# First batch reordered: queries load first, attention runs in a row, products of theta with the token weights' transposes between them

## The reference, cut to what matters

```
# attention without softmax: 8 batches, 8 heads, 576 tokens, head size 64
kv  = k^T v                                   # per head, 64 x 64
x   = rmsnorm(q @ kv) * g_norm                # -> [8, 576, 512], token-major
# first block
theta = x @ w_theta                           # 512 x 512
y   = w_tok_r @ (x*cos(theta)) + w_tok_i @ (x*sin(theta))    # 576 x 576 weights
u   = x + y
x2  = u + relu(u @ w_ch)
# second block
u2  = x2 + (relu(x2^T @ w_tok1) @ w_tok2)^T
out = u2 + relu(u2 @ w_ch1) @ w_ch2
```

## Time and profile before

| | us |
|---|---|
| median of 3 runs | 1176.14 (1175.67 to 1176.28) |
| profiled execution, device time | 1176.91 |
| its span in the profile | 1175.1 |
| PE busy | 1154.3 (98%) |
| DVE busy | 834.9 (71%) |
| ACT busy | 481.0 (41%) |
| POOL busy | 327.9 (28%) |

### The profile page before, as it was taken

One profiled execution on the slowest core, in us unless ns is written; L12 is line 12 of the kernel. 1 busy time (PEld: TensorE's weight loads), 2 busy tenths in 40 slices (PEclk: granted clock), 3 DMA queues, 4 the chain that ended last, 5 costly groups with the idle time before them and its releaser, 6 DMA issues.

```text
span 1175.1 us, 20563 instructions
## 1 busy us (share of the span) xinstructions
PE 1154.3 (98%) x7790; PEld 1116.7 (95%) x7790; DVE 834.9 (71%) x1243; ACT 481.0 (41%) x758; POOL 327.9 (28%) x210
## 2 busy tenths in 40 slices
PE   5999999999999999999999999999999999999998
PEld 5799999999999999999988999999999999999998
DVE  3968878686969687777557667667666786666664
ACT  3623425141424233334343555555556543333331
POOL 4462434444353534331552313214200000000000
PEclk9999999999999999999999999999999999999999
DMA  9714526160625330319997888666768999999983
GB/s 278 197 28 107 122 69 133 44 144 13 164 38 149 52 80 0 83 42 303 332 310 279 280 310 272 266 238 242 286 229 312 397 300 293 262 252 307 296 207 54
DMA packets 327383, 228.25 MB, mean 194 GB/s; under 512 B 231440, under 2 KB 295312, under 8 KB 326288
## 3 DMA queue, kind: packets, MB, share of 16 engines
q1 hardware_dynamic: 324912, 227.03, 63.3%
q10 hardware_dynamic: 2400, 0.30, 0.2%
HBM read 136.84 MB, written 92.80 MB: 195 GB/s over the span
## 4 chain that ended last, share of the span: by engine, by line
PE 86%; DMA 5%; DVE 3%; SPq 2%; issue 1%; POOL 1%; ACT 1%; DVEq 0%; ACTq 0%; POOLq 0%
PE bank L43 10%; PE bank L45 10%; PE bank L44 10%; PE bank L1377 10%; PE bank L1379 10%; PE bank L1378 10%; PE bank L367 6%; PE bank L373 6%; PE bank L368 6%; DMA u_scratch<-attention_u 3%; PE bank L312 3%; PE bank L326 1%; PE bank L282 1%; DMA attention_g<-g_scratch 1%; DVE attention_u L1268 1%
## 5 line engine op out<-in xcount | busy, mean ns | idle before, releaser
L367 PE MATMUL bank<-weights_tok,z_z 128*128 128x288 f32 x576 | 164.3, 300 | 0.3
L368 PE MATMUL bank<-weights_tok,z_z 128*128 128x288 f32 x576 | 161.2, 294 | 0.0
L373 PE MATMUL bank<-weights_tok,z_z 128*128 128x288 f32 x576 | 125.0, 295 | 0.8 <-POOL z_z L965 0.6
L367 PEld LDWEIGHTS bank<-weights_tok,z_z 128*128 128x128 f32 x576 | 108.1, 188 | 1.2 <-issue 1.1
L368 PEld LDWEIGHTS bank<-weights_tok,z_z 128*128 128x128 f32 x576 | 108.1, 188 | 0.0
L948 POOL TENSOR_TENSOR weights_rms_inverse<-weights_mean_squares,weights_minus_half 128x8 f32<-128x8 f32 x40 | 66.4, 1662 | 114.2 <-DVE weights_mean_squares L725 114.0
L373 PEld LDWEIGHTS bank<-weights_tok,z_z 128*128 128x128 f32 x576 | 92.5, 187 | 1.3 <-POOL z_z L965 0.8
L596 ACT ACTIVATE weights_x_channel_major<-attention_u 128x288 fp32r<-128x288 f32 x64 | 28.5, 446 | 139.0 <-DVE attention_u L792 139.0
L43 PE MATMUL bank<-weights_x_channel_major,weights_ch 128*128 128x288 f32 x256 | 77.4, 302 | 0.0
L963 POOL TENSOR_TENSOR z_z<-tokens_cos,z_z 128x512 fp32r<-128x512 f32 x24 | 31.9, 1329 | 159.8 <-ACT z_z L589 143.8
L45 PE MATMUL bank<-weights_x_channel_major,weights_ch 128*128 128x288 f32 x256 | 75.4, 294 | 0.0
(11 more groups left out here) (297 smaller groups left out, 3589.7 us busy)
## 6 DMA issues: line engine op xcount, KB each, us to landing
g_scratch<-attention_staged SPq DMA_DIRECT2D x36, 960.0 KB, 3.9
weights_g<-g_scratch SPq DMA_DIRECT2D x24, 1152.0 KB, 10.6
g_scratch<-attention_staged SPq DMA_DIRECT2D x36, 384.0 KB, 4.7
x_scratch<-attention_u SPq DMA_DIRECT2D x8, 1152.0 KB, 4.5
u_scratch<-attention_u SPq DMA_DIRECT2D x16, 576.0 KB, 7.6
weights_raw_u<-u_scratch SPq DMA_DIRECT2D x6, 1536.0 KB, 7.7
qkv_u_left<-u_scratch SPq DMA_DIRECT2D x12, 768.0 KB, 10.1
x_tokens_scratch<-z_x_turned SPq DMA_DIRECT2D x112, 72.0 KB, 2.0
```

The source lines that it names most:

```text
L367: pe.matmul(out, x, wtok[0][:, zt, hs], start=(i == 0), stop=False)
L368: pe.matmul(out, x, wtok[1][:, zt, hs], start=False, stop=False)
L373: mm = pe.matmul(tok_bank(b, g)[:, 0:HALF], z[1][:, zt, c * P:(c + 1) * P], wtok[0][:, zt, half * HALF:(half + 1) * HALF], start=False, st ...
```

## The change

It reorders the first batch on all five queues, and moves two things in phase b:

- SP loads all five query tiles right behind keys and values, then g_norm, theta's weights, the token weights, batch 1; the channel weights come last.
- PE transposes the identity 24 times into a spare bank before `kv(0)`.
- `attend` of batch 0 gets four banks (`out_bank`), and only its last tile waits for a `norm`. The five tiles run in a row with no `tok_weight` between.
- `theta(0, 0)` to `theta(0, 3)` run "by parts": hi·hi products wait for half the weights at a time, the next `x_transpose` follows, then the products with x's remainder, then with the weights' remainder. The `tok_weight` steps all come behind products of theta, two at a time from the second on; the last four use four banks (`ps_wt`). `kv(1)` comes ahead of the last `tok_weight`, and its copy moves from DVE to ACT.
- POOL's first `z_lo` waits for the last transposes of the token weights on PE instead of L872; that wait now stands ahead of its third tile.
- In phase b SP waits for both halves of the store of u2(n) before it loads x2(n+2), and ACT instead of SP issues `store_last_turned(1..3)`, at the end of its `batch(n)`.

```diff
+    ps_out_first = [*ps_out, ps_acc[0], ps_acc[1], ps_out[0]]
+    ps_wt = [ps_acc[i % 2] for i in range(9)] + [ps_out[0], ps_acc[2], ps_acc[1]]
+    def out_bank(n, j):
+        return ps_out_first[j] if isinstance(n, int) and n == 0 else ps_out[j % 2]
...
-        sp.dma_start(gn[:, :], g_norm...).then_inc(s_raw[1], DMA)
         for j in range(NT):
             load_query_tile(0, j, s_q0[j])
-            if j == 1:
-                load_tok(w_tok_r, raw_tok[0], s_raw[3])
+        sp.dma_start(gn[:, :], g_norm...).then_inc(s_raw[1], DMA)
         sp.dma_start(raw_theta[:, :, :], ...).then_inc(s_raw[0], DMA)
+        load_tok(w_tok_r, raw_tok[0], s_raw[3])
         load_tok(w_tok_i, raw_tok[1], s_raw[4])
-        sp.dma_start(raw_ch[:, :, :], ...).then_inc(s_raw[2], DMA)
         load_kv(1)
         sp.wait_ge(p_qt, NT)
         for j in range(NT):
             load_query_tile(1, j, s_q)
+        sp.dma_start(raw_ch[:, :, :], ...).then_inc(s_raw[2], DMA)
...
        def theta(b, j, by_parts=False):
...
-                    if x == 0:
-                        pe.wait_ge(*((a_whi, 2) if w == 0 else (d_wlo, 2)))
-                    else:
-                        pe.wait_ge(d_xlo, 1)
+                    if x == 1:
+                        pe.wait_ge(d_xlo, j + 1)
                     for c in range(NC):
+                        if x == 0 and c % 2 == 0:
+                            pe.wait_ge(*((a_whi, c // 2 + 1) if w == 0 else (d_wlo, c // 2 + 1)))
...
+                    if w == 0 and x == 0:
+                        x_transpose(b, j + 1)
...
     def tensor(pe, nxt):
...
+        pe.wait_ge(s_ident, 2)
+        for i in range(24):
+            pe.transpose(ps_acc[0][:, 0:P], ident[:, :], ident[:, :])
         pe.wait_ge(s_zero, 2)
         kv(0)
...
+        q_transpose(0, 2)
+        q_transpose(0, 3)
+        attend(0, 2)
+        q_transpose(0, 4)
+        attend(0, 3)
+        attend(0, 4)
         x_transpose(0, 0)
+        theta(0, 0, by_parts=True)
+        tok_weight(0)
+        theta(0, 1, by_parts=True)
+        tok_weight(1)
+        tok_weight(2)
+        theta(0, 2, by_parts=True)
+        tok_weight(3)
+        tok_weight(4)
+        theta(0, 3, by_parts=True)
+        tok_weight(5)
+        tok_weight(6)
+        theta(0, 4)
+        tok_weight(7)
...
+        tok_weight(10)
+        kv(1)
+        tok_weight(11)
+        q_transpose(1, 0)
...
     def scalar(act, nxt):
...
+        theta_weight_hi(0)
         x_hi(0, 0)
+        theta_weight_hi(1)
         squares(0, NT - 1)
...
     def vector(dve, nxt):
...
+        theta_weight_lo(0)
+        x_lo(0, 0)
+        theta_weight_lo(1)
         norm(0, 2)
+        x_lo(0, 1)
         mean_square(0, 4)
         norm(0, 3)
...
     def gpsimd(gp):
...
-                gp.wait_ge(d_wt, 2 * NT + 1)
+                gp.wait_ge(p_wt, 2 * (NT + 1))
             for j in range(NT):
+                if isinstance(b, int) and b == 0 and j == 2:
+                    gp.wait_ge(d_wt, 2 * NT + 1)
                 z_lo(b, j)
...
     def sync(sp, nxt):
...
             if n + 2 < B:
+                sp.wait_ge(s_st[1], DMA * (n + 1))
                 load(sp, n % 2, n + 2)
-            if 1 <= n < NC:
-                store_last_turned(sp, n)
...
         def batch(n):
...
+            if 1 <= n < NC:
+                store_last_turned(act, n)
```

More of the change, by code:

```diff
@@ L307, in attend @@
             pe.wait_ge(kv_placed, 4 * (n + 1))
-            wait(pe, d_xn, NT * n + max(j - 1, 0))
+            if isinstance(n, int) and n == 0:
+                if j == NT - 1:
+                    pe.wait_ge(d_xn, 1)
+            else:
+                wait(pe, d_xn, NT * n + max(j - 1, 0))
             if j == 1:
@@ L397, in token_mix_first_half @@
             for pair in range(NT):
+                if first and pair == NT - 1:
+                    pe.wait_ge(a_whi, 3)
+                    pe.wait_ge(d_wt, 2 * NT + 1)
                 token_mix_pair(b, pair, FIRST_HALF)
@@ L488, in body @@
                     theta(b, j)
-            if more:
+            if more and not first:
                 kv(b + 1)
-                if first:
-                    q_transpose(b + 1, 0)
             if first:
-                pe.wait_ge(a_whi, 3)
                 pe.wait_ge(a_wt, 2 * NT)
-                pe.wait_ge(d_wt, 2 * NT + 1)
+                pe.wait_ge(a_left, 4)
+                pe.wait_ge(d_wt, 2 * NT)
             if more:
@@ L953, in gain @@
             if j == 0:
+                gp.wait_ge(s_raw[1], DMA)
                 wait(gp, d_z, 2 * NT * n)
```

147 lines of the change are left out of this document (74 added, 73 removed).

## The result

The changed kernel takes 1184.22 us (median of 4 runs, 1182.87 to 1186.95) against 1176.21 for the kernel before beside it: 8 us more, ratio 1.0072, 95% interval 1.0051 to 1.0093. The profiled execution took 1182.87 us, its span 1181.1. The forecast was 1173.1.

What follows compares the result with a forecast made beforehand. The prediction took PE, busy 98% of the span, as the bound, so only its waits could be won. First batch -3.5 and phase b +0.5 gave -3.0 us on 1176.9, so 1173.9, or 1173.1 as median; range 1170.5 to 1177.5.

Steps and rivals of the forecast that it cites:

- Both terms of the sum: The first batch was forecast at -3.5 us and phase b at +0.5 us.
- the two signs: PE waiting for DVE by more than 1 us between 27 and 48 us, or phase b's waits past 3 us.
- Step "Phase b, ACT": Stores issued on ACT in phase b: four take 2.7 us; one `hidden_hi` comes late, costing +0.6 to +1.5 us.
- Rival 4: Phase b: ACT is held by store issue of 7 us, three `hidden_hi` late, +11.2 us, 1183.8 in all; chance 0.07.
- Step "Phase b, SP": Phase b's x2 loads wait for u2's store and run 3.9 us later, by itself hidden; bounds -1.3 to +3.5 us.
- Rival 3: Phase b: deferred x2 loads meet the token loads, +3.5 us, 1176.1 in all, no change; chance 0.17.
- Step "POOL": First batch: POOL's first `z_lo` starts 4.6 us earlier, and its last ends at 64.0 instead of 67.5 us.
- Rival 2: First batch: DVE becomes the bound, stretched 2 us by contention with POOL; gain only -1.5, 1175.1 in all; chance 0.17.
- The theta weights' arrival: First batch: theta's weights land 3.5 to 3.8 us earlier, at about 21.7 us; theta's first product starts at 23.4.
- the transposes lift the clock: Start of the kernel: 24 identity transposes raise PE's clock and save 0.5 us, with 0 as the other bound.
- the rule cited: Start of the kernel: transposes do not count as clock-gate activity as products do, so the 24 would lift nothing.

Runs made afterwards that it cites:

- e1: The changed kernel with phase b put back as before, so only the first batch is changed; 1.0013 of the kernel before.
- e2: The kernel before with only phase b's two edits (SP's wait, stores on ACT), first batch as before; 1.0045 of the kernel before.
- e17: The kernel before with only the stores of turned tiles moved to ACT at the end of the batch, no SP wait; 1.0023 of before.
- e7: The changed kernel without SP's wait ahead of the x2 loads, stores still on ACT; 1.0048 of the kernel before.
- e11: The kernel before with the stores on ACT behind the next batch's hidden Relus and token copies, no SP wait; 0.9989 of before (1175.42 us against 1176.48).
- e16: The kernel before with only SP's wait for u's store ahead of the x2 loads, stores still on SP; 1.0092 of before.
- e6: The changed kernel with ACT's stores moved one batch later, behind the hidden Relus and token copies, SP's wait kept; 1.0050 of the kernel before.
- e9: The kernel with the first batch changed and phase b as before, without the 24 identity transposes; 1.0022 of the kernel before.
- e15: The kernel of e14 without the 24 identity transposes; 1.0006 of the kernel before.
- e13: The kernel before with the 24 identity transposes at the start and nothing else; 1.0022 of before.
- e3: The changed kernel with the stores back on SP behind the x2 loads, SP's wait kept; 1.0116 of the kernel before.
- e5: The changed kernel with 36 spare products in PE's phase-b wait for `hidden_hi`; 1.0074 of the kernel before.
- e10: The kernel with the first batch changed and phase b as before, its first batch's last `z_lo` done by DVE; 1.0018 of the kernel before.
- e14: Changed kernel without SP's wait, ACT's stores behind next batch's Relus, last `z_lo` on DVE, channel weights' low part split between DVE and POOL; 1.0005 of before.
- e8: First batch changed, phase b as before, with POOL's first `z_lo` again waiting for DVE's last token weight; 1.0025 of the kernel before.

## Why the prediction was wrong

Both terms of the sum failed, by about as much. The first batch had -3.5 us and measured +1.5 (e1, interval 0.4 to 2.7); phase b had +0.5 and measured +5.3 (e2, 3.3 to 7.3). Of the two signs it named for being wrong, phase b's waits came (4.9 us, for a limit of 3), and a wait of PE for DVE of over 1 us between 27 and 48 us did not.

**Step "Phase b, ACT": four issues at 0.67 us each.** It put 2.7 us for four issues "where ACT's queue is empty", from six stores at the end of the kernel. In the changed kernel they took 6.74, in e2 7.32, in e17 6.66, in e7 5.68. Alone this costs 2.7 us (e17). The nearest row was the other one, 8.16 us for the same four stores at nearly the same moment on SP. Which queue issues them made little difference; the moment did: on ACT the same four took 3.5 us 7 us later (e11), and on SP 2.9 us 8 us later (e16). That the work of the DMA engines at that moment is what stretches them fits this, but no run isolates it. Rival 4 described the case, at a chance of 0.07 and a time of 1183.8. That this is near the measured 1184.22 is luck: it named three late `hidden_hi`, for 11.2 us, and only the first was late, and it kept the first batch's gain of 3.5. The groups of batches 2 and 3 took 4.6 and 2.0 us, behind their `hidden_hi` of that time, and held nothing that was due.

**The same step left the clock out.** A wait of 4.7 us was followed by slower products that cost 2.2 us. The prediction priced no wait's consequence for the clock anywhere; the first batch has it too.

**Step "Phase b, SP": "by itself that is hidden".** It is not. The wait alone costs 10.6 us with the stores on SP (e16), though it had the bounds -1.3 to +3.5. Two parts of the step were off. The x2 loads were to run 3.9 us later; they left 9.1 us later in e16 and 10.6 us later in the change. And "SP has the time" did not hold, since SP's queue, which kept the stores in e16, took 15.6 to 17.3 us a batch there. In the change itself this was partly covered: its residual waits were 0.2 us, since PE was late already. With the stores out of the way (e6) the wait costs 4 us or so. Rival 3 named the mechanism, x2 loads up against the token loads, and its price of 3.5 is about what e6 shows (sum 96.0 for 91.7). The Trainium skill (DMA: Bandwidth & Descriptors, Queues, rings and completion order) was cited for a dearer half of the range; no run here separates that rule from plain bandwidth.

**Step "POOL": `rotate(0, 3)` "at 49.6".** It started at 53.63, and the last lo products at 67.38 instead of 64.0. The walk took DVE's durations from a stretch in which POOL was waiting, and then placed the work beside POOL's. Of the 4.0 us, 3.0 are the three operations at 1.44, 1.78 and 1.85 us for 0.68, 0.68 and 0.75; DVE was 1 us late before them. Rival 2 had contention as its reason, but placed it at 28.9 to 51.5; it began at 48, with the very `z_lo` that the change brings forward. The Trainium skill (GPSIMD Engine Reference, Specifications) says that POOL's interfaces to SBUF are shared with DVE, with contention for DVE instructions that have two SBUF inputs or run in a 2-port perf mode. The rows agree on the two inputs: 0.68 against 1.77 us for the same operation, while the one of 57.03 that reads a PSUM bank kept its 0.67. An operation with one SBUF input was stretched as well, the TENSOR_SCALAR of `magnitude` (1.40 us for 64 rows at 60.29 beside POOL, 0.43 for 128 rows at 43.91); no row says in which mode it ran.

**What was right.** The theta weights' arrival and everything up to 47 us, to within 1 us, in the changed kernel's profile. In part that is luck: of the ten profiles with this start and the transposes, five began theta at 23.6 to 23.9 and five at 25.0 to 25.5. It was also right that the transposes lift the clock. On this point the rule cited from the Trainium skill (TensorE: Matmul & The Clock Gate, Part 4: PE-mode transpose) and the rows differ: behind 24 transposes and nothing else, 32 key products take 1.15 us, without them 1.97 to 1.98, in all profiles. The measurement decides. But the lift was worth nothing that could be measured in the new order (e9, e15) and less than 0 in the old one (e13), not 0.5.

**What stays open.** Why PE was back at the lower level at the query transposes in e3, e5, e10 and e14 and not in others, with the same instructions. The 24 transposes ahead took 4.2 to 4.4 us there (and in e1) and 4.7 to 5.4 in the others; no run tells what decides that. Why the keys landed late in e1. And which of its parts makes the four runs of the changed kernel spread over 4.1 us; that the clock falls in some executions and not in others would do it, but only profiled executions show it.

## What to carry to other kernels

Read an issue's price at the moment at which it will be issued: a row of the same transfer at the same time on the other queue is nearer than a row of an empty one, and nothing that is due soon may stand behind it on the engine. Before a wait is put ahead of a load, add up everything that stands behind it in the same queue, and compare it with the time of one batch. Before POOL and DVE are made to overlap, re-price every operation that has both inputs in SBUF as if the other were running. And a wait of PE can cost more than its length: here two waits of 1.2 and 1.4 us with little work between them were mostly followed by a slower clock worth another 1.6 to 2.7 us, so a reordering that leaves PE's total work alone but opens such a hole near its end can give back all that it won.

## What the runs showed of the hardware

- Transposes of the identity alone raise PE's clock: 32 products with 64 columns in 1.15 us behind them, 1.97 without.
- DVE and POOL: on DVE 128x512 with two SBUF inputs 0.68 us alone, 1.77 beside POOL; 64x512 0.68 alone, and 2.00 when it began inside an operation of POOL's, 0.55 us behind whose end it ended (e14). POOL's own 1.3 us alone, 1.6 to 1.8 beside DVE.
- Four stores of 72 KB in rows of 128 bytes: 5.7 to 8.2 us to issue on SP or ACT at 569 to 572 us, 2.9 to 3.5 us on either at 576 to 583 us (e16, e11).
- Clock at 0.5 for some us: behind waits of PE of 4.7, 4.3 and 4.2 us (the changed kernel, e2, e17); in 5 of 7 profiles behind waits of 1.24 and 1.40 us with 1.3 us of products between; in neither of two behind 1.24 and 1.86 us with 2.3 us between; in both of two behind one of 2.55 us (e14, e15); behind 2.87 (e13) and 2.93 us (e8).
- The length of a wait alone does not tell: in phase b the clock fell behind waits of 1.97, 2.37 (e3), 2.46 (e6) and 2.96 us (e16), and stayed at 1.00 behind 1.91 (e10), 2.10 (e7), 2.81 (e16) and 3.28 us (e3).
